# The first product of the second expert layer: eight block products against Strassen's seven

## The reference, cut to what is computed

```python
# 1. attention, 4 batches x 8 heads x 576 positions x 64: a pooled softmax (factor 4) plus a local band
x = (out_up + out_local) -> (2304, 512)
# 2. first expert layer: 512 -> 2048 -> 512
h = x @ w_in;  g = h * tanh(softplus(h));  x = g @ w_out
# 3. second expert layer: 512 -> 1024 -> 512
h = x @ w_in
e = exp(h - max(h));  sm = e / (sum(e) + 1e-9)
solu = h * sm
ln = (solu - mean(solu)) / sqrt(var(solu) + 1e-6) * g_ln
out = ln @ w_out
```

## Time and profile before

| | us |
|---|---|
| median of 3 runs | 723.61 (723.29 to 727.32) |
| the profiled execution | 726.61 |
| its span, first to last instruction | 724.8 |
| second layer on PE, from its first product to its last | 501.98 to 721.73 |

### The profile page before, as it was taken

The page is one execution under the profiler, slowest core; times in us unless marked ns, Lnnn a source line. Parts: engine busy times, 40 slices in busy tenths (PEclk is TensorE's granted clock), DMA queues, the critical chain, the costliest instruction groups (busy, mean ns, idle before and its releaser), DMA issues.

```text
span 724.8 us, 12338 instructions
## 1 busy us (share of the span) xinstructions
PE 696.6 (96%) x5152; PEld 640.5 (88%) x5152; DVE 326.6 (45%) x640; ACT 245.3 (34%) x525; POOL 93.1 (13%) x123
## 2 busy tenths in 40 slices
PE   5878889999999999999999999999999999999997
PEld 5767669999999999999999999999788888888886
DVE  7986976552233222322322332226754444444441
ACT  5866875332111211121121112116543434343432
POOL 5976930000000000000000000002000000000000
PEclk9998999999999999999999999999999999999999
DMA  8996882000000000000000000006000000000001
GB/s 232 244 250 192 232 293 106 1 0 1 1 1 1 1 0 1 1 1 1 0 1 1 1 1 1 0 1 232 0 30 15 29 15 30 15 29 15 30 15 44
DMA packets 24423, 37.50 MB, mean 52 GB/s; under 512 B 2480, under 2 KB 12720, under 8 KB 24368
## 3 DMA queue, kind: packets, MB, share of 16 engines
q1 hardware_dynamic: 24368, 36.71, 16.9%
HBM read 31.99 MB, written 4.72 MB: 51 GB/s over the span
## 4 chain that ended last, share of the span: by engine, by line
PE 79%; POOL 6%; DVE 5%; issue 5%; DMA 3%; ACT 1%; SPq 1%; POOLq 0%; DVEq 0%
PE psum L537 27%; PE psum L551 26%; PE psum L631 12%; PE psum L607 11%; POOL half_v L412 2%; PE psum L617 2%; POOL half_qk L399 2%; DMA v<-v_dram 1%; POOL vd L413 1%; POOL prob L420 1%; DVE wlo L1020 1%; POOL qd L402 1%; DMA kT<-kT_dram 1%; DVE wlo L1079 1%; DMA wraw<-w_dram 1%
## 5 line engine op out<-in xcount | busy, mean ns | idle before, releaser
L983 DVE CAST ghi<-g_sb 128x384 fp32r<-128x384 f32 x96 | 34.5, 360 | 260.9 <-PE psum L551 204.0
L725 ACT ACTIVATE g_sb<-psum 128x384 f32<-128x384 f32 x96 | 47.2, 492 | 302.0 <-PE psum L537 302.0
L537 PE MATMUL psum<-xhi,whi 128*128 128x384 f32 x384 | 129.5, 337 | 1.1 <-DVE wlo L949 0.8
L537 PE MATMUL psum<-xhi,wlo 128*128 128x384 f32 x384 | 129.0, 336 | 0.0
L551 PE MATMUL psum<-ghi,wlo 128*128 128x384 f32 x384 | 129.0, 336 | 0.0
L551 PE MATMUL psum<-ghi,whi 128*128 128x384 f32 x384 | 129.0, 336 | 0.0
L551 PE MATMUL psum<-glo,whi 128*128 128x384 f32 x384 | 129.0, 336 | 0.0
L537 PE MATMUL psum<-xlo,whi 128*128 128x384 f32 x384 | 129.0, 336 | 0.0
L537 PEld LDWEIGHTS psum<-xhi,whi 128*128 128x128 f32 x384 | 72.2, 188 | 2.2 <-issue 0.7
L537 PEld LDWEIGHTS psum<-xlo,whi 128*128 128x128 f32 x384 | 72.2, 188 | 0.0
L551 PEld LDWEIGHTS psum<-ghi,whi 128*128 128x128 f32 x384 | 72.2, 188 | 0.0
(11 more groups left out here) (95 smaller groups left out, 921.0 us busy)
## 6 DMA issues: line engine op xcount, KB each, us to landing
wraw<-w_dram SPq DMA_DIRECT2D x16, 512.0 KB, 6.8
qT<-qT_dram SPq DMA_DIRECT2D x16, 288.0 KB, 4.6
kT<-kT_dram SPq DMA_DIRECT2D x16, 288.0 KB, 6.2
v<-v_dram SPq DMA_DIRECT2D x16, 288.0 KB
out_dram<-ob SPq DMA_DIRECT2D x18, 256.0 KB, 2.0
vw<-v_dram SPq DMA_DIRECT2D x32, 128.0 KB, 4.3
wraw<-w_dram SPq DMA_DIRECT2D x4, 1024.0 KB, 8.5
vw<-v_dram SPq DMA_DIRECT2D x32, 32.0 KB, 4.3
```

The lines of the kernel that those rows point to most:

```text
L537: ins = nc.tensor.matmul(bank, a[:, w], b[:, kdx, :], start=(kdx == 0 and n == 0), stop=(kdx == KD - 1 and n == 2))
L725: nc.scalar.activation(g_sb[:, f % HR, :], psum[:, HB1 + f % HB, 0:N1], ACT.Mish).then_inc(g_ok, 1)
L983: nc.vector.tensor_copy(ghi[:, f % GR, :], g_sb[:, f % HR, :]).then_inc(ghi_ok, 1)
```

## The change

**Seven products for a tile pair.** Two tiles of 128 tokens are taken together. The 256 x 512 tokens A are cut into 2 x 2 blocks (two token tiles, two halves of the contraction), the 512 x 1024 weights B into 2 x 2 blocks of 256 x 512. Where eight block products gave the 2 x 2 blocks of h, now seven do (Winograd's form of Strassen's method): four sums of token blocks and four of weight blocks are formed ahead, and seven results are combined behind. `product(p, n)` is 2 blocks of the contraction x 3 matmuls = 6 matmuls of 512 columns (L746 of the changed kernel); a pair has 42 where it had 48.

**What comes with it.** POOL forms the sums of the token blocks (`token_sums`, 4 of 128x256 a pair) and the low parts of all seven token operands (`token_lows`, 7 of 128x256), ACT their high parts (`tokens_high`, 7 of 128x256) and a copy of the first product (`copy_p1`). DVE does the seven combinations of 128x512 (`add_p6`, `make_c11`, `add_p7`, `make_c22`, `add_p5`, `make_c21`, `make_c12`) and no token splits any more. The products 2, 4 and 6 share one PSUM bank (`BB`), so each waits until DVE has read the one before; products 5 and 7 share another.

**What is moved.** The first product's weights go into a buffer of their own (`raw2`) while the first layer still runs. In the first layer's last tile POOL forms the sums of the weight blocks and four of their low parts, ACT four high parts, and both prepare the tokens of pair 0. PE's list mixes the first four products of pair 0 between the last three outputs of layer one. The tiles 0 to 3 have an order of their own; from pair 2 on the order repeats.

```diff
+        AB, BB, T2B = (2, 6), 0, 4
...
+            sp.wait_ge(added, T1 * KD)
+            sp.dma_start(raw2[:].rearrange("p k c -> p (k c)"), w2_d[:, 0:IN2]).then_inc(ld_w2in, 16)
             for c in range(W2C):
+                sp.wait_ge(y_mm, LAST + 2 * (OUT2 - IN1) // WB + 2 * (c + 1))
...
+            pool.wait_ge(ld_w2in, 16)
+            pool.wait_ge(y_mm, LAST + 2)
+            b12 = b_block(3)
+            nc.gpsimd.tensor_tensor(t1[:], b12, b_block(0), ALU.subtract).then_inc(t_ok, 1)
...
+            for n in range(EARLY):
+                pool.wait_ge(w2hi_ok, n + 1)
+                nc.gpsimd.tensor_tensor(w2_block(wlo, n), b_block(n), w2_block(whi, n).bitcast(F32), ALU.subtract)\
...
+            pool.wait_ge(y_mm, LAST + 8)
+            token_sums(0)
+            token_lows(0)
+            token_sums(1)
+
+            pool.wait_ge(y_mm, T1 * F1)
+            token_lows(1)
+            token_sums(2)
+            root(0)
+            root(1)
+            token_lows(2)
+            root(2)
+            root(3)
+            for p in range(2, PAIRS2):
+                if p + 1 < PAIRS2:
+                    token_sums(p + 1)
+                    token_lows(p + 1)
+                root(2 * p)
+                root(2 * p + 1)
...
+            def product(p, n):
+                bank = psum[:, (AB[p % 2], BB, AB[p % 2], BB, AB[p % 2] + 1, BB, AB[p % 2] + 1)[n], :]
+                pe.wait_ge(ylo_ok, NPR * p + n + 1)
...
+                elif n == 2:
+                    pe.wait_ge(p1_ok, p + 1)
+                elif n == 3:
+                    pe.wait_ge(p16_ok, p + 1)
+                elif n == 5:
+                    pe.wait_ge(p167_ok, p + 1)
+                else:
+                    pe.wait_ge(p165_ok, p + 1)
+                for k in range(KH):
+                    w = slice(WJ[n] * WB + k * C2, WJ[n] * WB + (k + 1) * C2)
+                    for m, (a, b) in enumerate(((yhi, whi), (ylo, whi), (yhi, wlo))):
+                        ins = nc.tensor.matmul(bank, a[p % 2][:, n, k, :], b[:, w],
...
+            def turn2(t):
+                par = t % 2
                 pe.wait_ge(ln_ok, t + 1)
                 wait(pe, llo_ok, t * 2)
...
+            output(T1, -3)
+            product(0, 0)
+            product(0, 1)
+            output(T1, -2)
+            product(0, 2)
+            product(0, 3)
+            output(T1, -1)
+            for n in range(EARLY, NPR):
+                product(0, n)
+            for n in range(NPR):
+                product(1, n)
+            pe.wait_ge(y_ev, T1 + 1)
+            for t in range(2):
+                turn2(t)
+            for t in range(2):
+                output2(t, 0)
+                output2(t, 1)
+            for p in range(2, PAIRS2):
+                product(p, 0)
+                product(p, 1)
+                turn2(2 * p - 2)
+                product(p, 2)
+                product(p, 3)
+                product(p, 4)
+                turn2(2 * p - 1)
+                product(p, 5)
+                product(p, 6)
+                output2(2 * p - 2, 0)
+                output2(2 * p - 2, 1)
+                output2(2 * p - 1, 0)
+                if p == PAIRS2 - 1:
+                    turn2(T2 - 2)
+                output2(2 * p - 1, 1)
...
+            for n in range(EARLY, NPR):
+                weights_two_in(n)
+            copy_p1(0)
+            nc.scalar.preload_act_table_set("natural_log_exp_and_others")
+            tokens_high(1, 0, NPR)
+            act.wait_ge(ld_g, 16)
+            for c in range(F2 - 2):
+                weights_two_out(c)
+            evict_last(KD // 2)
+            evict_last(0)
+            copy_p1(1)
...
+            def make_c22(p):
+                dve.wait_ge(h2_mm, NPR * p + 5)
+                dve.wait_ge(p167_ok, p + 1)
+                nc.vector.tensor_tensor(hrow[:, C2:FF2], psum[:, AB[p % 2] + 1, :], p167[:], ALU.add)\
+                  .then_inc(c22_ok, 1)
+
+            def add_p5(p):
+                nc.vector.tensor_tensor(p165[:], psum[:, AB[p % 2] + 1, :], p16[:], ALU.add).then_inc(p165_ok, 1)
```

More of the change, by code:

```diff
@@ L63 @@
 EPS_LN = 1e-6
-W2C = 2 * KD
-WC = 2 * KD * FF2 // W2C
+NPR = 7
+KH = KD // 2
+C2 = FF2 // 2
+PAIRS2 = T2 // 2
+WJ = (0, 2, 4, 6, 1, 3, 5)
+EARLY = 4
+W2C = F2 // 2
+OUT2 = 12 * WB
+LAST = (T1 - 1) * F1
 def first_query(i, jp):
@@ L154, in program @@
         g_sb = sb("g_sb", [P, HR, N1])
+        od_at = top[0]
         od = sb("od", [P, KD, TOK // POOLF])
@@ L587, in _ @@
                 output(t, F1 - LAG)
[L588 to L610, removed]
@@ L1059, in layernorm @@
                                         ALU.add, ALU.mult).then_inc(ln_ok, 1)
-            def tile_two(it, last=False):
-                for par in range(2):
-                    t = it * 2 + par
-                    if not (last and par == 1):
-                        split_y(t + 1, 1 - par)
-                    if par == 1 or not (it == 1):
-                        low2(t - 2, par)
-                    softmax_max(t, par)
-                    solu(t, par)
-                    if last and par == 1:
-                        low2(t - 1, 0)
-                    layernorm(t, par)
@@ L1075, in _ @@
[L1075 to L1082 removed]
+            for n in range(EARLY, NPR):
+                low_in(n)
+            add_p6(0)
+            for c in range(3):
@@ L1083, in _ @@
                 low_out(c)
-            softmax_max(0, 0)
-            for c in range(F2 - 2, F2):
+            make_c11(0)
+            add_p7(0)
+            for c in range(3, F2 - 2):
                 low_out(c)
-            solu(0, 0)
-            split_y(2, 0)
-            layernorm(0, 0)
-            softmax_max(1, 1)
-            solu(1, 1)
-            low2(0, 0)
-            layernorm(1, 1)
-            tile_two(1)
-            for it in range(2, T2 // 2 - 1):
-                tile_two(it)
@@ L1097, in _ @@
-            tile_two(T2 // 2 - 1, True)
-            low2(T2 - 1, 1)
+            make_c22(0)
+            add_p5(0)
+            make_c21(0)
+            make_c12(0)
+            softmax_max(0)
+            softmax_max(1)
+            add_p6(1)
+            solu(0)
+            make_c11(1)
+            add_p7(1)
+            solu(1)
+            make_c22(1)
+            add_p5(1)
+            layernorm(0)
+            make_c21(1)
+            layernorm(1)
+            make_c12(1)
+            low_out(F2 - 2)
@@ new lines, in _ @@
+            low_out(F2 - 1)
+            low2(0)
+            low2(1)
+            for t in range(2, 4):
+                softmax_max(t)
+            for t in range(2, 4):
+                solu(t)
+            for t in range(2, 4):
+                layernorm(t)
+            for p in range(2, PAIRS2):
+                add_p6(p)
+                low2(2 * p - 2)
+                make_c11(p)
+                add_p7(p)
+                make_c22(p)
+                add_p5(p)
+                low2(2 * p - 1)
+                make_c21(p)
+                make_c12(p)
+                for t in range(2 * p, 2 * p + 2):
+                    softmax_max(t)
+                for t in range(2 * p, 2 * p + 2):
+                    solu(t)
+                for t in range(2 * p, 2 * p + 2):
+                    layernorm(t)
@@ L1102 @@
+            low2(T2 - 2)
+            low2(T2 - 1)
 def kernel(**inputs):
```

361 lines of the change are left out of this document (227 added, 134 removed).

## The result

| | runs | median us (least to greatest) | ratio to before, 95% interval |
|---|---|---|---|
| before | 20 | 727.63 (723.29 to 733.19) | |
| changed | 20 | 723.67 (719.70 to 728.28) | 0.9949, [0.9929, 0.9970] |

The change makes the kernel faster by 0.5% (0.3 to 0.7%), 4.0 us between the medians.

The account below looks back on a forecast made before the run. PE was taken to bound the second layer, with little waiting to remove. Matmuls saved (-12.6), added waits (+7.35) and low clock (+1.7) sum to -3.6 us, off the 723.61 median: 720.0 us, range 715.5 to 726.5.

Parts of the forecast that it names:

- I keep the price of each: PE's second layer: operand shapes and weight loads stay, so each 512-column matmul still costs 0.2335 us.
- The saving: PE's second layer: 9 pairs x 6 matmuls x 0.2335 us, 12.6 us less, all on PE's path.
- The repeating order: Pairs 2 to 8 of the second layer: DVE, POOL and ACT keep up, so PE has no added wait.
- The last tile of layer one: POOL's wide operations there delay DVE by 6.3 us over four steps, but this is covered and costs nothing.
- The handover: From layer one to the second layer, and at the tail: waits of 9.65 us against 2.3 before, +7.35 us.
- The clock: Behind the 5.7 us gap at turn2(1), PE runs 3.4 us at half clock, costing 1.7 us; bounds 0 and 3.3.
- the slower rival: Handover gaps of 2.0, 1.45 and 5.7 us are each followed by 6.6 us at 1.2 GHz: 727 us; chance 0.14.
- Taken off the median, the forecast is 720.0: Whole kernel: the sum of -3.6 us is counted from the earlier median of 723.61 us, giving 720.0 us.
- A difference is hardly told from none: Whole kernel: differences below 1% of the median, 7.2 us, count as the same; chance of the same 0.83.
- Layernorm is held too: Handover rival: layernorm 1, ahead of turn2(1), waits for one POOL token_lows operation, 0.74 us more, 720.7 us; chance 0.20.
- a handover that hides: Handover rival: DVE's list runs 5 us shorter, only 2 to 4 us of waits, no low clock: 712 us; chance 0.10.
- a wait in every pair: Repeating-order rival: combinations of 1.4 us make product 7 late by 0.8 us in 7 pairs: 726 us; chance 0.07.

Follow-up runs that it names:

- e4: The changed kernel with the six matmuls of product 7 issued twice in pairs 2 to 8; 734.26 us in one run, stage 233.6 us.
- e5: The changed kernel with odd pairs' split-token buffers and what follows them 448 bytes further in SBUF; 716.72 us in one run, stage 221.7 us.
- e7: The kernel before with two small constants moved, so both layers' token buffers and what follows lie 64 bytes nearer; 724.38 us, ratio 0.9952.
- e2: The changed kernel with low2 of tile 0 moved on DVE directly behind layernorm of tile 1; 718.35 us, ratio 0.9855, stage 219.2 us.
- v2: The kernel with low2(0) first, plus four output weights' low parts ahead of add_p6(0) on DVE and their feeding ahead of copy_p1(0) on ACT; 716.59 us, ratio 0.9846.
- e1: The changed kernel with 24 unused matmuls of 512 columns between turn2 of tiles 0 and 1; 721.51 us, ratio 0.9917, stage 222.2 us.
- e6: The kernel before with both layers' token and hidden-row buffers and what follows them 64 bytes further in SBUF; 734.04 us, ratio 1.0113.

## Why the prediction was right and wrong

In the order of its steps; the sum is of the stage, -4.73. Three steps failed: "I keep the price of each", which left out 1.9 us; the term for the clock, 1.7 where it was 2.2; and what was made of the sum, the base of 720.0 and the reading that a gain of this size is no change.

- **The saving, -12.6: right in kind** (54 matmuls fewer, no wait from 545 to 700; e4 puts back six a pair and the stage grows by 9.3). **The sentence "I keep the price of each" failed.** The change moves the tokens of even pairs and `lhi` to another place, and a pair takes 22.64 us (outputs from 559.13 to 581.77) or 22.44 (to the next, at 604.21), 22.54 on average, not the 22.76 of 90 matmuls at 0.2335 and two transposes. Over nine pairs that is -1.9 which the sum does not have. e5 and e7 show that the place alone changes the price; with equal places the change is worth 3.2 us, near the -3.6 forecast.
- **The repeating order, no wait: right.** The unknown price, an addition that writes PSUM, is 0.70 us.
- **The last tile of layer one, nothing: right.** DVE was held there (its cast to `ghi`, L1159, took up to 2622 ns, 413 on average over the span; before, 360 on average), and layer one still took 398.4.
- **The handover, waits of 9.65: right, each within 0.6.** 1.4 for 2.0, 1.4 for 1.45, 5.6 for 5.7, 0.3 for 0.3; the 0.2 at `turn2(0)` does not show as a wait. They add up to 8.7; the first operation behind each took 0.2 to 0.3 longer than it does in a stream (1.64 for a product behind its wait, where half of 2.74 is 1.37), four times, which makes it about 9.6 against 9.65. The walk had DVE's list as the cause, and changes of that list take 2.9 off the 5.6 (e2) and, with ACT's list changed to feed it, all of the first 1.4 (v2). The 1.4 at product 7 of pair 1 was there in every run of the changed kernels (1.3 to 1.4), and no experiment touched its cause.
- **The clock, 1.7: right in kind, too small.** One stretch of 6.7 us at 0.50, 2.2 to 2.3 us (e1). I took the length from the gap nearest in size; the other row there, 6.6 us, was the right one. Its half, 3.3, would have been too much, because the low stretch began 1.94 us before the wait ended, and only what PE did in it cost time: half of 4.76 is 2.4. The shorter gaps of 1.4, and of 2.7 in e2, left the clock at 1.00, which rules out the slower rival.
- **The sum:** -12.6 + (9.6 - 2.3) + 2.2 - 1.9 = -5.0 against -4.73 measured; the 0.3 between them was not traced. That -3.6 came so near is in part luck: a term of -1.9 was missing and one of 1.7 was 0.5 too small, and the two errors have opposite signs.
- **"Taken off the median, the forecast is 720.0" failed**, and with it the number. Against the profiled execution's own 726.61 the sum gave 723.0, and the changed one measured 723.73; against the median of 20 runs, 724.0. Three runs between 723.29 and 727.32 do not say where the median lies when runs spread over 10 us; the profiled execution was the better base of the two, and it stood in the text. But each of these two figures hangs on one run, and layer one began 1.85 us later in the changed one (99.16 against 97.31), so that they lie this close is luck too.
- **"A difference is hardly told from none" below 1%: failed.** With 20 runs a side the interval is 0.2% either way, and 0.5% is a gain, not no change. My likeliest forecast was this gain, and I counted it as the same.
- **Layernorm is held too (chance 0.20): true, at 0.4 us, not 0.74.** Layernorm 1 took 1.20 beside a subtraction, 0.81 alone. The Trainium skill ("SBUF — State Buffer", section "Who interferes with whom") has it that a `tensor_scalar` can enter a 2-port mode and can then contend with GpSimd; the 1.20 agrees, though no view here names the mode. The same section of the Trainium skill has it that an operation of DVE with two SBUF inputs contends with a GpSimd instruction that reads SBUF and not with one that only writes it. The traces agree: 3.04 for three splits beside subtractions, 2.06 beside memsets.

The other rivals, a handover that hides, a wait in every pair, a stalled layer one, did not happen.

## What to carry to other kernels

A saving that moves buffers is two changes: look at the time between like operations before and after, and try the old kernel with its buffers moved before the method gets the credit. At the step from one stage to the next, walk the list of the engine that feeds the bound one; here one line moved in such a list was worth more (5.2 us, 2.3 of it the clock that no longer fell) than the whole change as it was made (4.7). And forecast the difference that the sum gives: the base that it was taken from was off by 4.0 us, the sum by 1.1.

## What the runs showed of the hardware that was not expected

- Matmuls of 512 columns with the same instructions follow each other at 0.227, 0.2325 or 0.2333 us as the tokens' buffer lies 0, 128 or 64 bytes, within 512, from the start of the weights' (5.44, 5.58 and 5.60 for 24). In layer one, where tokens are the moving operand, 12 of 384 columns take 2.08 at 0 and 64 and 2.11 at 128. In e5, e6 and e7 the buffers behind the one that was moved were moved with it. Three places were tried; what the rule is between them, and why, stays open.
- One DVE operation with one SBUF input was held by seven memsets of POOL in a row until the last of them (2.28 for 0.81, its end 0.55 behind the seventh), not only by the one that ran when it began. This was seen once.
- A PE gap of 2.7 us behind the products of pair 1 and `turn2(0)` left the clock at 1.00 (e2), where one of 2.19 between attention's 64x64 matmuls was followed by 0.50.
